# A bound on the loads in flight in a chain of attention and two gated feed-forward layers

## The reference

```python
# 1: attention with decay, 8 heads of 64, in blocks of 64 tokens (the kernel takes blocks of 128)
for b in range(nb):
    intra = (qb @ kb.T * Dmask) @ vb
    inter = (qb * lam_pow) @ kv_state
    out[:, :, sl] = intra + inter
    kv_state = lam_block * kv_state + (kb * rev_pow).T @ vb
# 2: feed-forward, d_ff = 1024, x_prev is x shifted by one token
xk = mu_k * x + (1.0 - mu_k) * x_prev
xr = mu_r * x + (1.0 - mu_r) * x_prev
x = sigmoid(xr @ w_r) * (relu(xk @ w_k) ** 2 @ w_v)
# 3: gate from a causal convolution over 5 tokens
gate = sigmoid(sum(conv_w[k] * shifted(x, 4 - k) for k in range(5)))
out = (gate * (x @ w_val)) @ w_out
```

## Time and profile before

| | us |
|---|---|
| time, median of 3 runs | 276.83 (275.75 to 277.29) |
| the profiled execution | 276.0 |
| its span in the trace | 274.2 |
| TensorE busy (matmuls) | 269.9 |
| VectorE busy | 166.0 |
| ScalarE busy | 125.4 |
| GpSimd busy | 23.6 |

### The profile page before, as it was taken

The page is one execution under the profiler, slowest core; times in us unless marked ns, Lnnn a source line. Parts: engine busy times, 40 slices in busy tenths (PEclk is TensorE's granted clock), DMA queues, the critical chain, the costliest instruction groups (busy, mean ns, idle before and its releaser), DMA issues.

```text
span 274.2 us, 4270 instructions
## 1 busy us (share of the span) xinstructions
PE 269.9 (98%) x1746; PEld 226.3 (83%) x1746; DVE 166.0 (61%) x258; ACT 125.4 (46%) x223; POOL 23.6 (9%) x25
## 2 busy tenths in 40 slices
PE   8999999999999999999999999999999999999996
PEld 7889977888888888888888888888888888888886
DVE  5866999998581125465885553429969599325000
ACT  2237788977582124365721234748217306412121
POOL 1667750000000000000000000000000000000000
PEclk9999999999999999999999999999999999999999
DMA  7999996000000000000000000530000000310323
GB/s 215 408 410 406 406 407 253 0 0 2 0 0 0 2 0 0 0 2 0 0 0 2 2 0 0 174 134 0 0 0 2 0 0 0 117 38 0 115 82 111
DMA packets 7506, 22.57 MB, mean 82 GB/s; under 512 B 960, under 2 KB 1216, under 8 KB 7488
## 3 DMA queue, kind: packets, MB, share of 16 engines
q1 hardware_dynamic: 7488, 22.31, 21.4%
HBM read 19.16 MB, written 3.15 MB: 81 GB/s over the span
## 4 chain that ended last, share of the span: by engine, by line
PE 96%; DVE 2%; DMA 1%; issue 0%; ACT 0%
PE ps L717 28%; PE ps L719 28%; PE ps L718 28%; PE ps L799 4%; PE ps L733 4%; PE ps L783 2%; PE ps L761 2%; DMA prm<-in_prm 1%; DVE dec L608 1%; DVE pT L508 0%; DVE qdec L589 0%; ACT out_sb L414 0%
## 5 line engine op out<-in xcount | busy, mean ns | idle before, releaser
L717 PE MATMUL ps<-xk_h,wk_h 128*128 128x512 f32 x96 | 37.5, 391 | 0.0
L718 PE MATMUL ps<-xk_l,wk_h 128*128 128x512 f32 x96 | 37.4, 389 | 0.0
L719 PE MATMUL ps<-xk_h,wk_l 128*128 128x512 f32 x96 | 37.4, 389 | 0.0
L717 PE MATMUL ps<-kk_h,wv_h 128*128 128x512 f32 x96 | 37.3, 389 | 0.0
L718 PE MATMUL ps<-kk_l,wv_h 128*128 128x512 f32 x96 | 37.3, 389 | 0.0
L719 PE MATMUL ps<-kk_h,wv_l 128*128 128x512 f32 x96 | 37.3, 389 | 0.0
L571 DVE SCALAR_TENSOR_TENSOR gate<-x,prm,gate 128x512 f32<-128x512 f32 x48 | 32.6, 748 | 0.0
L547 DVE SCALAR_TENSOR_TENSOR kk_f<-ps,ring 128x512 f32<-128x512 f32 x24 | 16.6, 691 | 24.1 <-ACT ring L367 24.1
L384 ACT ACTIVATE gate<-x,prm 128x512 f32<-128x512 f32 x12 | 8.7, 725 | 43.2 <-DVE x L557 43.2
L367 ACT ACTIVATE ring<-ps 128x512 f32<-128x512 f32 x24 | 14.3, 597 | 26.7 <-PE ps L719 26.7
L717 PEld LDWEIGHTS ps<-xk_h,wk_h 128*128 128x128 f32 x96 | 18.0, 188 | 4.0 <-issue 0.3
(11 more groups left out here) (74 smaller groups left out, 487.5 us busy)
## 6 DMA issues: line engine op xcount, KB each, us to landing
qk<-in_qk SPq DMA_DIRECT2D x12, 512.0 KB, 11.3
kv<-in_kv SPq DMA_DIRECT2D x9, 512.0 KB, 12.8
out<-out_sb SPq DMA_DIRECT2D x11, 256.0 KB, 2.0
wk_raw<-in_w_k SPq DMA_DIRECT2D x4, 512.0 KB, 14.2
wv_raw<-in_w_v SPq DMA_DIRECT2D x4, 512.0 KB, 12.5
wr_raw<-in_w_r SPq DMA_DIRECT2D x2, 512.0 KB, 15.0
w_raw<-in_w_val SPq DMA_DIRECT2D x2, 512.0 KB, 4.4
w_raw<-in_w_out SPq DMA_DIRECT2D x2, 512.0 KB, 6.9
```

Of the source, the lines that this page charges most:

```text
L717: nc.tensor.matmul(to, left(0), right(0), start=(i == 0), stop=False)
L718: nc.tensor.matmul(to, left(0), right(1), start=False, stop=False)
L719: done = nc.tensor.matmul(to, left(1), right(0), start=False, stop=(i == last))
```

## The change

SyncE gets a wait ahead of 26 of its loads, from kv(1) to the second piece of w_r. Each wait is for the landing of an earlier load, the third one ahead, and the fourth for some in the first pairs. The semaphores are those that were there. The order of the loads, their sizes and all other engines' programs stay as they were. The lines below SyncE's program move down in the file by up to 31.

```diff
+            def qk_landed(n):
+
+                sp.wait_ge(qk_here[n % IN_BUFS], 16 * (n // IN_BUFS + 1))
+
+            def kv_landed(n):
+
+                sp.wait_ge(kv_here[n % IN_BUFS], 16 * (n // IN_BUFS + 1))
+
             sp.dma_start(prm[:, :], prm_in).then_inc(prm_here, 16)
             load_qk(0)
             load_qk(1)
             sp.dma_start(kv[0][:, 1, :], v0_in).then_inc(kv_here[0], 16)
             load_qk(2)
+            qk_landed(0)
             load_kv(1)
+            qk_landed(1)
             load_qk(3)
+            kv_landed(0)
             load_kv(2)
+            qk_landed(2)
             load_qk(4)
+            kv_landed(1)
             load_kv(3)
+            qk_landed(3)
             load_qk(5)
+            kv_landed(2)
             load_kv(4)
+            qk_landed(4)
             load_kv(5)
             for p in range(3, NP - 1):
+                qk_landed(2 * p - 1)
                 load_qk(2 * p)
+                kv_landed(2 * p - 2)
                 load_qk(2 * p + 1)
+                kv_landed(2 * p - 1)
                 load_kv(2 * p)
+                qk_landed(2 * p)
                 load_kv(2 * p + 1)
+            qk_landed(NCH - 3)
             load_qk(NCH - 2)
+            kv_landed(NCH - 4)
             load_qk(NCH - 1)
+            kv_landed(NCH - 3)
             load_weight(wk_raw, w_k, 0, wk_here)
+            qk_landed(NCH - 2)
             load_kv(NCH - 2)
+            qk_landed(NCH - 1)
             load_kv(NCH - 1)
-            for i in range(1, 4):
-                load_weight(wk_raw, w_k, i, wk_here)
-            for i in range(2):
-                load_weight(wr_raw, w_r, i, wr_here)
+            sp.wait_ge(wk_here[0], 16)
+            load_weight(wk_raw, w_k, 1, wk_here)
+            kv_landed(NCH - 2)
+            load_weight(wk_raw, w_k, 2, wk_here)
+            kv_landed(NCH - 1)
+            load_weight(wk_raw, w_k, 3, wk_here)
+            sp.wait_ge(wk_here[1], 16)
+            load_weight(wr_raw, w_r, 0, wr_here)
+            sp.wait_ge(wk_here[2], 16)
+            load_weight(wr_raw, w_r, 1, wr_here)
```

## The result

The changed kernel takes 282.25 us (median; 280.68 to 282.66), the kernel before 276.76 in the runs beside it. The ratio is 1.020, with a 95% interval of 1.017 to 1.023: 5.5 us slower. The forecast was 277.0 us, in a range of 275.7 to 278.6, with 0.14 for slower. It was wrong.

What follows compares the result with a forecast made beforehand. TensorE was taken to bound the kernel, with loads landing just in time. The waits would cost it 0 to 0.3 us, taken as 0.2: 276.83 + 0.2 = 277.0 us, range 275.7 to 278.6.

Steps and rivals of the forecast that it cites:

- What bounds the kernel: Attention stage: TensorE sets the pace, busy 269.9 of 274.2 us, with loads fast enough at 406 to 410 GB/s.
- the slack: Time between a load's landing and TensorE's need: 0.2 us for qk(5), 0.5 for qk(7), 1.5 for qk(11).
- the upper bound of a round: Attention loads: from one landing to that of the load it releases at most 4.0 us, costing TensorE 0.3 us.
- The lower bound: Attention loads: 2.6 us of delay nearly hidden by 2.56 us of data in two loads on the way, cost 0.
- The slow rival: Attention loads: a round outlasts the window and the stream thins out; 278.2 to 280.6 us; chance 0.14.
- The row of 5.0 us: Second piece of w_val, queued behind another load: 5.0 us to landing; such a round would cost TensorE 3.8 us.
- The small gain: Attention loads: a shorter queue lets each land sooner, at most 0.61 us gained, 276.2 us; chance 0.10.
- What should have shown it: Signs of a wrong forecast: stage rate of 350 GB/s or less, TensorE gaps naming a DMA, stage ending over 1 us later.

Runs made afterwards that it cites:

- the thin kernel without waits: Kernel before, no waits added, with TensorE's 8 attention matmuls per group merged into 2 or 4 with more columns (products not right): 275.9 us.

## Why the prediction was wrong

**What bounds the kernel** was read rightly. TensorE set the pace, the loads came just in time, and the slack was what the rows said: qk(5) and qk(7), with 0.2 and 0.5 us, are among the first that TensorE waits for, and the late start of the first hidden tile comes from the loads ahead of it, all but the 1.1 us of the longer instruction on VectorE.

**The step that failed** is the upper bound of a round: "A full round is then at most 3.9 + 0.1 = 4.0 us, as these two rows include the start on an idle path." Both rows, qk(0) and the first piece of w_val, are of loads for which all 16 DMA engines start together: their 16 updates lie 0.5 and 0.6 us apart. They hold the cold start, but not the distance between the engines that a stream builds up, 1.7 us at qk(5) in the same trace. With all of them together and nothing queued a round is even shorter, 3.2 us. In the stream it is 5.3 to 5.5. What I missed is that a landing is one time for 16 engines. No row of the page tells how far they are apart, but the trace of before does, in the updates of each load's semaphore. I compared the round with the data that three loads hold, 3.84 us, as if every engine still had two loads left at the landing. At qk(5)'s landing most of them had nothing left to do.

**The lower bound** rested on the same picture, that 2.6 us of delay would be hidden by 2.56 us of data, and was no bound of what could happen either. The kernel needs five on the way to be free of loss, 5.1 us of data at the end of the wait.

**The slow rival was right** in the outcome and in how a long round reaches TensorE, but not in why a round is long: it spoke of the way of a load through the queue, and that way alone is 3.2 us. It said that a round longer than the window costs TensorE from 4.4 us on, 2.2 us at 4.6 and 3.8 at 5.0, which is 0.4 us for each 0.1; carried on to 5.4 that gives 5.4 us, and 5.5 were measured. So close a match is luck. The rival's 5.4 us are all lost by qk(11), which would land some 6.8 us late, and it landed 5.5 late (37.74 instead of 32.19). In the runs 3.6 of the 5.5 us come from the waits up to the first piece of w_k, 1.9 from the weights, which the rival had at nothing, and 1.1 us of the first hidden tile's delay is the longer instruction on VectorE. What was wrong besides was its chance of 0.14, and the argument against it, "both rows near it say 3.9, and they pay for a cold start". The row of 5.0 us, which I set aside because it queued behind another, was the nearest one: in the changed kernel every load queues behind others.

**w_r and w_v** were said to have the first hidden tiles in front of them. With the later pieces of w_k they cost 1.9 us: w_r's second piece landed at 54.2 instead of 41.7 us, 12 us late and not 2.3.

**The small gain** from a shorter queue did not show. In the profile after, prm landed after 1.7 us instead of 2.8, and the first attend started at 7.91 instead of 8.33. But the thin kernel without waits had prm as early (1.6 us), so this isn't the waits' doing, and with five and six on the way the time is that of before.

**What should have shown it** did: a rate under 350 GB/s in the stage, gaps at scores(7) and scores(11)'s group and at the first hidden tile that name a DMA or what hangs on it, and a stage that ends over 1 us later.

## What to carry to other kernels

A wait for a landing is a wait for the slowest of 16 DMA engines; if it gates the next issue, the data on the way must cover the isolated round and the distance between the engines. Here that took five loads of 512 KB (2.6 MB) and not the two and a half that the isolated round asks for. A bound taken from loads that start on idle engines is no bound for a stream; the nearest row is one of a load that queues. Where a kernel must limit what is on the way, deepen the limit until the moved GB/s stop rising, and only then look at the time.

## What was unexpected of the hardware

- The 16 DMA engines are apart in a stream: first and last update of one load's semaphore came 1.7 us apart in the kernel before, and 0.46 us (median) with one load on the way.
- In a round with a 16 KB fetch of TensorE's instructions one DMA engine ended late: with one load on the way, the other 15 updates came 2.0 us before the last, and the round took 5.3 instead of 3.1 us. That the fetch was the reason is likely but not shown, as three rounds with a fetch stayed under 4 us.
- The low part of w_k's first piece took VectorE 2.29 us when GpSimd's qd ran beside it, and 1.21 us when not.
- Where DMA engines run out of work, their rate for busy time is lower: 346 against 397 GB/s for a full share.
- With one load on the way the granted TensorE clock fell. The stretch from 10 to 40 us has a mean of 0.78, between the two levels of 1.2 and 2.4 GHz (0.5 and 1); with two on the way it was 0.89, with three 1.00. It was at the lower level from 27.0 to 40.7 us. Between 9 and 27 us TensorE had waited for loads five times, 1.4 to 3.0 us each, and a group of scores that took 1.16 us before took 2.08 at 28.15:

```profile
10.00:40.00 30.00, 14.43 (x216) 12.23 (x220) 6.86 (x13) 4.21 (x13) 6.68 (x7) 0.78 0.40 141
```
